# The first feature block of the first tile, computed in groups of 128 tokens between the pieces of the attention's lead-in

## The chip, the cores and the metric

The kernel runs on one core of one Trainium2 chip. The metric is the device time of one execution in microseconds (us). The kernel before took 1025.87 us, the median of 3 runs (1025.23 to 1028.19). A difference of a few tenths of a per cent is what such a measurement can tell from no change.

## The reference

All data is fp32. Three stages follow each other.

```python
# 1. attention in chunks of 32 tokens, 8 heads of 64, 768 tokens, 4 batches
for c in range(nc):
    k_full = np.concatenate([mem_k, k_ctx], axis=2)      # 8 memory + 16 left + 32 + 8 right = 64 keys
    scores = scale * np.matmul(q_c, k_full.transpose(0, 1, 3, 2))
    a = np.exp(scores - max); a = a / (sum(a) + 1e-09)
    out[:, :, c_start:c_end] = np.matmul(a, v_full)
x = out.transpose(0, 2, 1, 3).reshape(3072, 512)
# 2. first MLP: the largest of three projections, then one back
h = np.maximum(np.maximum(x @ w1, x @ w2), x @ w3)      # 512 -> 768
x = h @ w_out
# 3. second MLP
h = x @ w_in                                             # 512 -> 2048
g = np.where(h >= 1, h, np.where(h <= -1, 0.0, (h + 1) ** 2 / 4))
return g @ w_out2
```

## The kernel before

The 3072 tokens are cut into 8 tiles of 384 tokens (`TT`), and a tile into 3 groups of 128 (`GPT`). Phase A does attention and the first MLP, phase B the second MLP. Each engine has its own program, written out by hand; the order of work on an engine is the order of its program, and semaphores tie the engines together.

**Matrix products of the MLPs.** Each operand is split in two fp32r parts, `hi` and `lo`. The helper `three` (L399 to L404) issues three matmuls for one product: w_hi by x_hi (L402), w_lo by x_hi (L403), w_hi by x_lo (L404). Each loads its own weights of 128x128 and streams the tokens; in the first MLP that is 384 columns. In `layer1(t, a, f, w)` (L406) a feature block f of 128 features is made for one of the three weight matrices w, over 4 blocks of 128 input features (`KD`): 12 matmuls of 384 columns into the PSUM bank `mlp[w]`. A tile has 6 feature blocks, each for w = 0, 1, 2. ScalarE copies the bank of w = 0 (`h_first`), VectorE takes the maximum with the banks of w = 1 and w = 2 (`h_second`, `h_third`), and the result is split again (`h_high`, `h_low`).

**Attention of a group.** TensorE makes the scores (`scores`, L371, 64 small fp32 matmuls). VectorE takes the row maximum and subtracts it (`softmax_shift`), ScalarE takes the exponential, VectorE makes sums, reciprocal and product (`softmax_scale`), TensorE transposes the probabilities (`transposes`, L378, 4 matmuls with 128x128 weights and 128 columns), ScalarE copies them out (`transposed`), TensorE multiplies by V (`weighted_v`, L395, 64 small fp32 matmuls), ScalarE and VectorE split the result into `x_hi` and `x_lo` (`x_high`, `x_low`; semaphore `x_lo_done`).

**The lead-in.** Inside a loop the attention of the next tile's three groups is set between the feature blocks of this tile. Before the first tile there is nothing to set it between: TensorE does the attention of groups 0 to 2 alone (L472 to L486) and then begins `tile_a(0, ...)`, whose first `layer1` waits for the `x_lo` of all three groups (L457). After the 12 matmuls of w = 0 the scores of group 3 are made (L460), then w = 1 and w = 2 follow. In the first three groups the exponentials go to the banks `mlp[0]` to `mlp[2]` (`first_exponent`, L546), which are free again once `prob_done` has counted the group.

**Weights of phase A** come in 8 pieces of 768 KB through three staging buffers (`load_wa`, L227). ScalarE copies a piece to its `hi` part (`w_high`); the `lo` part is made by GpSimd for pieces 0 and 1 (L332 to L335, semaphore `wa_first`) and by VectorE for the others (`w_low`). A staging buffer is loaded again when its piece is split (L230). Piece f holds the weights of feature block f for w = 0, 1, 2. In ScalarE's program the split of piece 1 stands behind the `x_high` of group 2 (L608, L609).

Of the kernel before, what the change touches and what calls it, by code (L numbers as in the profile page):

```python
# [11 lines left out]
P = 128  # L12
# [15 lines left out]
GPT = TT // P  # L28
TOKENS = B * S
TILES = TOKENS // TT  # L30
KD, KF1, KF2 = DM // P, F1 // P, F2 // P
# [13 lines left out]
def build_attention_and_two_mlps(nc, qk_l, v_l, w123, w_out1, w_in2, w_out2, out):  # L45
# [8 lines left out]
    with ExitStack() as ctx:  # L54
        def psum(name, cols):
            return ctx.enter_context(nc.psum_tensor(name, [P, cols], F32))

        def sem(name):
            return ctx.enter_context(nc.semaphore(name))

        def sbuf(where, name, shape, dt=F32):
            return where.enter_context(nc.sbuf_tensor(name, [P, *shape], dt))
# [22 lines left out]
        w123_hi = sbuf(phase_a, "w123_hi", [KF1, 3 * KD, P], F32R)  # L85
        w123_lo = sbuf(phase_a, "w123_lo", [KF1, 3 * KD, P], F32R)
# [29 lines left out]
        x_hi, x_lo = (x0_hi, x1_hi), (x0_lo, x1_lo)  # L116
        y_hi, y_lo = (y0_hi, y1_hi), (y0_lo, y1_lo)

        mlp = [psum(f"mlp{i}", BANK)[:, :] for i in range(MLP_BANKS - 1)]
# [29 lines left out]
        sum_done, den_done, rec_done, prob_done = sem("sum_done"), sem("den_done"), sem("rec_done"), sem("prob_done")  # L149
        trans_done, prob_t_done = sem("trans_done"), sem("prob_t_done")  # L150
        attn_done, x_hi_done, x_lo_done = sem("attn_done"), sem("x_hi_done"), sem("x_lo_done")
        stage_a_in = [sem(f"stage_a_in{i}") for i in range(A_STAGES)]
        wa_hi_done, wa_first, wa_split = sem("wa_hi_done"), sem("wa_first"), sem("wa_split")
        mlp_done = sem("mlp_done")
# [23 lines left out]
        def h_wait(e, s, t, f):  # L178

            e.wait_ge(s, KF1 * t + f + 1)  # L180
# [5 lines left out]
        def weights_split(e, n):  # L186

            if n < A_FIRST:
                e.wait_ge(wa_first, n + 1)
            else:  # L190
                e.wait_ge(wa_split, n - A_FIRST + 1)
# [164 lines left out]
        def _(pe):  # L356
            def scores_ready(n, j, uses):

                pe.wait_ge(qk_in[j], 16 * (uses + 1))
                if not isinstance(n, int) or n:  # L360
                    pe.wait_ge(sub_done, n)

            def scores(j):

                q, k = q_of(j), k_of(j)
                for i in range(HALF_HEADS):
                    for c in range(CPG):
                        part = slice(c * CHUNK, (c + 1) * CHUNK)
                        for r in range(2):
                            rows = slice(r * D, (r + 1) * D)  # L370
                            last = pe.matmul(scores_v[part, r, i], q[rows, i, part], k[rows, i, c], start=True, stop=True)  # L371
                last.then_inc(scores_done, 1)

            def transposes(n, slot):

                pe.wait_ge(prob_done, n + 1)
                for m in range(HALF_HEADS):
                    last = pe.transpose(trans_v[:, m], prob[:, slot, 2 * m:2 * m + 2], ident[:, :])  # L378
                last.then_inc(trans_done, 1)

            def weights_ready(n, j, uses):

                pe.wait_ge(v_in[j], 16 * (uses + 1))
                pe.wait_ge(prob_t_done, n + 1)
                if not isinstance(n, int) or n:
                    pe.wait_ge(x_lo_done, n)

            def weighted_v(j):

                for m in range(2):  # L390
                    for c in range(CPG):
                        for r in range(2):
                            for i in range(2):
                                rows = slice(i * D, (i + 1) * D)
                                last = pe.matmul(attn_o[r * D:(r + 1) * D, i, m, c], v_raw[rows, j, 2 * m + r, c],  # L395
                                                 prob_t[rows, 2 * m + r, c], start=True, stop=True)
                last.then_inc(attn_done, 1)

            def three(out_ap, ab, first, last):  # L399

                a_hi, a_lo, b_hi, b_lo = ab
                pe.matmul(out_ap, a_hi, b_hi, start=first, stop=False)  # L402
                pe.matmul(out_ap, a_lo, b_hi, start=False, stop=False)  # L403
                return pe.matmul(out_ap, a_hi, b_lo, start=False, stop=last)  # L404

            def layer1(t, a, f, w, ahead=None):  # L406
                bank = mlp[w]
                if f:

                    h_wait(pe, (h_part_done, h_max2_done, h_max3_done)[w], t, f - 1)  # L410
                elif w < 2:

                    pe.wait_ge(y_copied, KD * t + 3 + w)
                if isinstance(t, int) and t == 0 and w == 0:
                    weights_split(pe, f)
                for k in range(KD):
                    if ahead is not None and k == KD - 1:
                        ahead()
                    last = three(bank[:, 0:TT], (w123_hi[:, f, KD * w + k], w123_lo[:, f, KD * w + k],
                                                 x_hi[a][:, k], x_lo[a][:, k]), k == 0, k == KD - 1)  # L420
                last.then_inc(mlp_done, 1)

            def layer2(t, a, d):
                bank = mlp[L2_BANK[d]]
                if d == 0:
                    if isinstance(t, int) and t == 0:
                        weights_split(pe, A_PIECES - 1)
                    h_wait(pe, h_max2_done, t, KF1 - 1)
                if d == KD - 1:
                    pe.wait_ge(y_copied, KD * (t + 1) + 1)  # L430
                for f in range(KF1):

                    if d == 0 and f in (0, KF1 - 1):
                        h_wait(pe, h_lo_done, t, KF1 - 2 if f == 0 else f)
                    wc = slice(f * DM + d * P, f * DM + (d + 1) * P)
                    last = three(bank[:, 0:TT], (w_out1_hi[:, wc], w_out1_lo[:, wc], h_hi[:, f], h_lo[:, f]),
                                 f == 0, f == KF1 - 1)
                last.then_inc(mlp_done, 1)

            def tile_a(t, a, attention, first=False):  # L440

                n0 = GPT * (t + 1)
                for f in range(KF1):
                    j, r = divmod(f, 2)

                    def ahead():
                        weights_ready(n0 + j, j, t + 1)
                        if j + 1 < GPT:
                            scores_ready(n0 + j + 1, j + 1, t + 1)

                    if attention and f == 0:
                        scores_ready(n0, 0, t + 1)
                    if attention and r == 0 and j:
                        weighted_v(j - 1)
                        scores(j)
                    if f == 0:
                        pe.wait_ge(x_lo_done, GPT * (t + 1))  # L457
                    layer1(t, a, f, 0)
                    if attention and f == 0:
                        scores(0)  # L460
                    if attention and r:
                        transposes(n0 + j, (a + 1 + j) % 2)
                    layer1(t, a, f, 1)
                    layer1(t, a, f, 2, ahead if attention and r else None)
                if attention:
                    weighted_v(GPT - 1)
                for d in range(KD):
                    layer2(t, a, d)
# [12 lines left out]
            transposes(1, 1)  # L481
            weights_ready(1, 1, 0)
            weighted_v(1)
            transposes(2, 0)
            weights_ready(2, 2, 0)
            weighted_v(2)  # L486
            tile_a(0, 0, True, True)
            with pe.Fori(0, B - 1) as b:
                tile_a(2 * b + 1, 1, True)
                tile_a(2 * b + 2, 0, True)  # L490
# [45 lines left out]
        def _(act):  # L536
            def copy(o, i):
                return act.activation(o, i, ACT.Copy)  # L538
# [11 lines left out]
            def w_high(n):  # L550
                act.wait_ge(stage_a_in[n % A_STAGES], 16 * (n // A_STAGES + 1))
                copy(first_weights(n)[0], stage_of(n)).then_inc(wa_hi_done, 1)

            def transposed(n):

                act.wait_ge(trans_done, n + 1)
                if not isinstance(n, int) or n:
                    act.wait_ge(attn_done, n)
                copy(prob_t[:, :, :, :], trans_c).then_inc(prob_t_done, 1)

            def x_high(n, x, j):
                act.wait_ge(attn_done, n + 1)
                copy(x_of(x_hi[x], j), attn_x).then_inc(x_hi_done, 1)
# [41 lines left out]
            transposed(1)  # L605
            x_high(1, 0, 1)
            transposed(2)
            x_high(2, 0, 2)  # L608
            w_high(1)  # L609
            tile_a(0, 0, range(A_FIRST, A_PIECES))  # L610
            with act.Fori(0, B - 1) as b:
                tile_a(2 * b + 1, 1)
# [246 lines left out]
```

## Time and profile before

| | |
|---|---|
| median of 3 runs | 1025.87 us (1025.23 to 1028.19) |
| the profiled execution, its time | 1025.81 us |
| the profiled execution, its span | 1024.0 us |
| TensorE busy (PE) | 1004.9 us, 98% of the span |
| VectorE, ScalarE, GpSimd busy | 412.6, 302.3, 48.9 us |
| first 25.6 us of the span (first slice of 40) | PE busy five tenths, DMA engines eight tenths |

The span runs from the first to the last instruction of the profiled execution; its time has 1.81 us more, which lies outside of the span. PE stands for the matmuls, PEld for the weight loads, which overlap them. The profile models the end of a matmul, so the step from the start of one to the start of the next says what it costs. The chain of waits is followed back from the last instruction to whatever released each one.

### The profile page before, as it was taken

What the parts mean: (1) busy time and instruction counts of PE and PEld (TensorE: products, weight loads), DVE (VectorE), ACT (ScalarE), POOL (GpSimd) and SP (SyncE); (2) the same over time, 40 slices, a digit from 0 to 9 for tenths busy, and PEclk for the clock granted to TensorE, in tenths of its full rate; (3) what the DMA queues carried; (4) which work ended last, traced back from release to release, by engine and by line L of the source; (5) the groups of instructions that cost most, each with busy time, mean ns of one, the idle gap of its engine ahead of it and who ended that gap; (6) DMA issues with size and microseconds to landing.
All of it is one profiled execution on the core that took longest, in us unless ns stands there. A gap on an engine that the chain in (4) does not pass through costs nothing.

```text
span 1024.0 us, 19464 instructions
## 1 busy us (share of the span) xinstructions
PE 1004.9 (98%) x8160; PEld 940.8 (92%) x8160; DVE 412.6 (40%) x757; ACT 302.3 (30%) x543; POOL 48.9 (5%) x44
## 2 busy tenths in 40 slices
PE   5999999999999999999999999999999999999998
PEld 4999999999999999999999999999999899999997
DVE  4552424143342524224543444434434344344343
ACT  3342222222221212244333323333233233332322
POOL 1100000000000000054500000000000000000000
PEclk9999999999999999999999999999999999999999
DMA  8452223122222310055300000010000000000000
GB/s 360 166 186 69 98 84 105 53 84 89 98 73 65 104 52 2 24 159 163 109 32 31 1 31 31 8 54 0 31 31 0 31 31 31 31 0 0 31 0 31
DMA packets 21950, 65.96 MB, mean 64 GB/s; under 512 B 2432, under 2 KB 6528, under 8 KB 21888
## 3 DMA queue, kind: packets, MB, share of 16 engines
q1 hardware_dynamic: 21888, 65.02, 18.4%
q8 instruction: 53, 0.87, 0.4%
q14 instruction: 9, 0.07, 0.0%
HBM read 52.43 MB, written 12.58 MB: 63 GB/s over the span
## 4 chain that ended last, share of the span: by engine, by line
PE 98%; issue 1%; DMA 0%; DVE 0%; ACT 0%
PE mlp L402 20%; PE mlp L404 20%; PE mlp L403 20%; PE scores_ps L404 6%; PE scores_ps L403 6%; PE scores_ps L402 6%; PE trans_ps L403 3%; PE trans_ps L404 3%; PE trans_ps L402 3%; PE attn_ps L395 3%; PE attn_ps L404 2%; PE attn_ps L402 2%; PE attn_ps L403 2%; PE scores_ps L371 2%; PE trans_ps L378 1%
## 5 line engine op out<-in xcount | busy, mean ns | idle before, releaser
L402 PE MATMUL mlp<-x_hi,w_hi 128*128 128x384 f32 x576 | 197.6, 343 | 3.7 <-ACT y_stage L538 2.1
L404 PE MATMUL mlp<-x_lo,w_hi 128*128 128x384 f32 x576 | 193.6, 336 | 0.0
L403 PE MATMUL mlp<-x_hi,w_lo 128*128 128x384 f32 x576 | 193.3, 336 | 0.0
L657 ACT ACTIVATE squared<-clamped,half_col 128x384 f32<-128x384 f32 x128 | 78.9, 617 | 257.5 <-DVE clamped L804 257.5
L402 PE MATMUL mlp<-y_hi,w_in_hi 128*128 128x384 f32 x384 | 129.2, 336 | 1.5 <-issue 1.5
L404 PE MATMUL mlp<-y_lo,w_in_hi 128*128 128x384 f32 x384 | 129.3, 337 | 0.0
L403 PE MATMUL mlp<-y_hi,w_in_lo 128*128 128x384 f32 x384 | 128.8, 336 | 0.0
L402 PEld LDWEIGHTS mlp<-x_hi,w_hi 128*128 128x128 f32 x576 | 108.7, 189 | 6.4 <-ACT y_stage L538 2.7
L403 PEld LDWEIGHTS mlp<-x_hi,w_lo 128*128 128x128 f32 x576 | 108.8, 189 | 0.0
L404 PEld LDWEIGHTS mlp<-x_lo,w_hi 128*128 128x128 f32 x576 | 108.7, 189 | 0.0
L808 DVE TENSOR_TENSOR g_lo<-g_f,g_hi 128x384 fp32r<-128x384 f32 x128 | 73.3, 573 | 81.6 <-ACT g_hi L538 81.6
L404 PE MATMUL scores_ps<-w_out_lo,g_hi 128*128 128x512 f32 x256 | 101.4, 396 | 0.0
L403 PE MATMUL scores_ps<-w_out_hi,g_lo 128*128 128x512 f32 x256 | 100.9, 394 | 0.0
L402 PE MATMUL scores_ps<-w_out_hi,g_hi 128*128 128x512 f32 x256 | 99.5, 389 | 0.0
L804 DVE TENSOR_SCALAR clamped<-mlp 128x384 f32<-128x384 f32 x96 | 53.4, 556 | 113.9 <-PE mlp L404 113.9
L538 ACT ACTIVATE g_hi<-g_f 128x384 fp32r<-128x384 f32 x128 | 67.3, 526 | 85.3 <-DVE g_f L806 85.3
L806 DVE TENSOR_TENSOR g_f<-squared,mlp 128x384 f32<-128x384 f32 x96 | 53.2, 555 | 65.6 <-ACT squared L657 65.6
L402 PEld LDWEIGHTS mlp<-y_hi,w_in_hi 128*128 128x128 f32 x384 | 72.1, 188 | 5.2 <-issue 1.8
L538 ACT ACTIVATE h_hi<-h_max 128x384 fp32r<-128x384 f32 x48 | 25.2, 524 | 173.8 <-DVE h_max L732 173.8
L403 PEld LDWEIGHTS mlp<-y_hi,w_in_lo 128*128 128x128 f32 x384 | 72.1, 188 | 3.4
L404 PEld LDWEIGHTS mlp<-y_lo,w_in_hi 128*128 128x128 f32 x384 | 72.0, 188 | 0.0
L726 DVE TENSOR_TENSOR h_max<-h_part,mlp 128x384 f32<-128x384 f32 x48 | 26.6, 554 | 112.4 <-PE mlp L404 112.4
(77 smaller groups left out, 1401.0 us busy)
## 6 DMA issues: line engine op xcount, KB each, us to landing
qk_raw<-qk_l SPq DMA_DIRECT2D x24, 768.0 KB, 4.8
v_raw<-v_l SPq DMA_DIRECT2D x24, 512.0 KB, 5.5
y_scratch<-y_stage SPq DMA_DIRECT2D x32, 192.0 KB, 1.9
y_raw<-y_scratch SPq DMA_DIRECT2D x8, 768.0 KB, 4.2
out<-out_stage SPq DMA_DIRECT2D x24, 256.0 KB, 2.0
stage_b<-w_in SPq DMA_DIRECT2D x16, 256.0 KB, 2.9
stage_b<-w_out SPq DMA_DIRECT2D x16, 256.0 KB, 2.8
stage_a<-w SPq DMA_DIRECT2D x4, 768.0 KB, 6.9
```

The lines of the kernel that those rows point to most:

```text
L371: last = pe.matmul(scores_v[part, r, i], q[rows, i, part], k[rows, i, c], start=True, stop=True)
L378: last = pe.transpose(trans_v[:, m], prob[:, slot, 2 * m:2 * m + 2], ident[:, :])
L395: last = pe.matmul(attn_o[r * D:(r + 1) * D, i, m, c], v_raw[rows, j, 2 * m + r, c], prob_t[rows, 2 * m + r, c], start=True, stop=True)
L402: pe.matmul(out_ap, a_hi, b_hi, start=first, stop=False)
L403: pe.matmul(out_ap, a_lo, b_hi, start=False, stop=False)
L404: return pe.matmul(out_ap, a_hi, b_lo, start=False, stop=last)
L538: return act.activation(o, i, ACT.Copy)
L657: act.activation(squared[:, f % 2], clamped[:, f % 2], ACT.Square, bias=half_col[:, 0:1], scale=0.5).then_inc(square_done, 1)
L726: dve.tensor_tensor(h_max[:, f % 2], h_part[:, :], mlp[1][:, 0:TT], ALU.max).then_inc(h_max2_done, 1)
L804: dve.tensor_scalar(clamped[:, f % 2], h, -1.0, 1.0, ALU.max, ALU.min).then_inc(clamp_done, 1)
L806: dve.tensor_tensor(g_f32[:, f % 2], squared[:, f % 2], h, ALU.max).then_inc(g_done, 1)
L808: dve.tensor_tensor(g_lo[:, f % G_RING], g_f32[:, f % 2], g_hi[:, f % G_RING].bitcast(F32), ALU.subtract).then_inc(g_split, 1)
```

## The change

A new helper `first_block(w, j)` computes feature block 0 of tile 0 for weight matrix w and for the 128 tokens of group j alone: the same 12 matmuls, with 128 columns each. The nine calls take the place of the three `layer1` of f = 0, which are left out of the first tile. Two of them are placed around the transposes of group 2, one behind the `weighted_v` of group 2, and six after that, with the scores of group 3 behind `first_block(0, 2)`. Each w = 0 call waits for the `x_lo` of its own group. In ScalarE's program the split of piece 1 is moved ahead of the `x_high` of group 2.

```diff
+            def first_block(w, j):
+
+                if w == 0:
+                    pe.wait_ge(x_lo_done, j + 1)
+                if j == 0:
+                    if w == 0:
+                        weights_split(pe, 0)
+                    pe.wait_ge(prob_done, w + 1)
+                tok = slice(j * P, (j + 1) * P)
+                for k in range(KD):
+                    last = three(mlp[w][:, tok], (w123_hi[:, 0, KD * w + k], w123_lo[:, 0, KD * w + k],
+                                                  x_hi[0][:, k, tok], x_lo[0][:, k, tok]), k == 0, k == KD - 1)
+                if j == GPT - 1:
+                    last.then_inc(mlp_done, 1)
...
+                    if first and f == 0:
+                        continue
...
             weighted_v(1)
+            first_block(0, 0)
             transposes(2, 0)
+            first_block(1, 0)
             weights_ready(2, 2, 0)
             weighted_v(2)
+            first_block(2, 0)
+            for w in range(3):
+                first_block(w, 1)
+            scores_ready(3, 0, 1)
+            first_block(0, 2)
+            scores(0)
+            first_block(1, 2)
+            first_block(2, 2)
             tile_a(0, 0, True, True)
...
             transposed(2)
+            w_high(1)
             x_high(2, 0, 2)
-            w_high(1)
             tile_a(0, 0, range(A_FIRST, A_PIECES))
```

## Rows read from the trace of the kernel before

**Rows 1.** The page: busy time of the engines, granted clock by slices, the chain by engine.

```profile
PE 1004.9 (98%) x8160; PEld 940.8 (92%) x8160; DVE 412.6 (40%) x757; ACT 302.3 (30%) x543; POOL 48.9 (5%) x44
...
PEclk9999999999999999999999999999999999999999
...
PE 98%; issue 1%; DMA 0%; DVE 0%; ACT 0%
```

**Rows 2.** Timeline of PE, 17 to 25.3 us: start, us, engine, line, operation, count, idle before.

```profile
19.31 1.11 PE L378 MATMUL trans_ps<-ident,prob 128*128 128x128 f32 x4
21.15 1.93 PE L395 MATMUL attn_ps<-prob_t,v_raw 64*64 64x32 f32 x64 [0.73 <-ACT prob_t L538]
24.67 0.66 PE L402 MATMUL mlp<-x_hi,w_hi 128*128 128x384 f32 x1 [1.59 <-issue]
25.13 0.52 PE L403 MATMUL mlp<-x_hi,w_lo 128*128 128x384 f32 x1
```

**Rows 3.** Timeline of PE, 28 to 30.6 us.

```profile
28.33 0.52 PE L404 MATMUL mlp<-x_lo,w_hi 128*128 128x384 f32 x1
28.78 1.19 PE L371 MATMUL scores_ps<-qk_raw 64*32 64x64 f32 x64
29.90 0.45 PE L402 MATMUL mlp<-x_hi,w_hi 128*128 128x384 f32 x1
30.18 0.34 PE L403 MATMUL mlp<-x_hi,w_lo 128*128 128x384 f32 x1
```

**Rows 4.** PE in narrow windows inside the transposes at 19.3 and 36.25 us.

```profile
19.31 0.69 PE L378 MATMUL trans_ps<-ident,prob 128*128 128x128 f32 x2
...
19.31 0.90 PE L378 MATMUL trans_ps<-ident,prob 128*128 128x128 f32 x3
...
36.25 0.38 PE L378 MATMUL trans_ps<-ident,prob 128*128 128x128 f32 x2
...
36.25 0.49 PE L378 MATMUL trans_ps<-ident,prob 128*128 128x128 f32 x3
```

**Rows 5.** Timeline of PE at 500 us: matmuls of 384 and 512 columns.

```profile
500.34 0.33 PE L404 MATMUL mlp<-y_lo,w_in_hi 128*128 128x384 f32 x1
500.52 0.39 PE L402 MATMUL scores_ps<-w_out_hi,g_hi 128*128 128x512 f32 x1
500.75 0.40 PE L403 MATMUL scores_ps<-w_out_hi,g_lo 128*128 128x512 f32 x1
```

**Rows 6.** Timeline of weight loads (PEld) at 24.6 and 29.9 us.

```profile
24.64 0.29 PEld L402 LDWEIGHTS mlp<-x_hi,w_hi 128*128 128x128 f32 x1 [1.70 <-issue]
24.81 0.33 PEld L403 LDWEIGHTS mlp<-x_hi,w_lo 128*128 128x128 f32 x1
...
29.90 0.19 PEld L402 LDWEIGHTS mlp<-x_hi,w_hi 128*128 128x128 f32 x1 [0.17 <-issue]
30.00 0.19 PEld L403 LDWEIGHTS mlp<-x_hi,w_lo 128*128 128x128 f32 x1
```

**Rows 7.** Timeline of ScalarE, 20 to 26 us.

```profile
20.46 0.60 ACT L538 ACTIVATE prob_t<-trans_ps 128x512 f32<-128x512 f32 x1 [0.43 <-PE trans_ps L378]
23.63 1.48 ACT L538 ACTIVATE w_hi<-stage_a 128x1536 fp32r<-128x1536 f32 x1
```

**Rows 8.** Timeline of GpSimd, and of VectorE up to the first feature block.

```profile
14.46 3.44 POOL L335 TENSOR_TENSOR w_lo<-stage_a,w_hi 128x1536 fp32r<-128x1536 f32 x1 [12.99 <-ACT w_hi L538]
25.19 3.46 POOL L335 TENSOR_TENSOR w_lo<-stage_a,w_hi 128x1536 fp32r<-128x1536 f32 x1 [7.28 <-ACT w_hi L538]
...
23.77 0.69 DVE L716 TENSOR_TENSOR x_lo<-attn_ps,x_hi 128x512 fp32r<-128x512 f32 x1 [3.02 <-ACT x_hi L538]
```

**Rows 9.** Timeline of VectorE, 30 to 36 us: the softmax of group 3, piece 2.

```profile
30.73 0.69 DVE L698 TENSOR_TENSOR score<-scores_ps,row_max 128x512 f32<-128x512 f32 x1
32.29 0.55 DVE L726 TENSOR_TENSOR h_max<-h_part,mlp 128x384 f32<-128x384 f32 x1 [0.87 <-PE mlp L404]
33.92 0.69 DVE L711 TENSOR_TENSOR prob<-prob,row_rec 128x512 f32<-128x512 f32 x1
```

## The prediction

> **What bounds the kernel now.** I read the page first: TensorE (PE) is busy 98% of the span, the others 40% and less, and 98% of the chain of waits is PE's own work [rows 1]. So the end moves by whatever PE's program gets longer or shorter, as long as nothing new makes it wait. Then I read the timeline of PE where the change is. Until 24.67 us PE does the attention of three groups, with two holes: 0.73 us before the sums of group 2, which wait for ScalarE's copy, and 1.59 us before the first layer, where the profile says only "issue" but the x_lo of group 2 is being made, which ends at 24.46 us [rows 2, 8]. From 24.67 us on PE streams without a hole worth naming. These two holes, 2.3 us, are all that the change can fill with waiting time.
>
> The third thing to see is the rate. In the first 12 matmuls of 384 columns a step is (28.33 - 25.13) / 10 = 0.320 us, which is 384 columns at 1.2 GHz. From 30.18 us to the transposes at 36.25 us there are 35 such matmuls (11, 12 and 12), so a step is 6.07 / 35 = 0.173 us, and it is about that at 500 us too [rows 2 to 5]. So PE is on its low level up to some point between 28.33 and 29.90 us and on its high one (2.4 GHz) after. The granted clock on the page reads full in every slice [rows 1]; it doesn't show this, and the steps decide. The rise came at most 5.2 us after the first 384-column matmul. The attention before it, over 15 us of small fp32 matmuls and transposes, had not raised it.
>
> **The change part by part.** Removed: 36 matmuls of 384 columns, 12 on the low level (3.84 us) and 24 on the high one (24 x 0.173 = 4.15 us). Added: 108 matmuls of 128 columns, each with its own load of 128x128 weights. The columns in all are the same; the weight loads are three times as many. All hangs on what a pair of load and matmul costs at 128 columns, and no fp32r pair of this size is in the trace.
>
> From below: 512 columns take 0.23 us a step, 384 take 0.173, so cost is in proportion to columns, and 128 would be 0.058 us on the high level and 0.107 on the low one, if loads stay hidden [rows 2, 3, 5]. From above: a pair costs no more than the 384-column one, 0.173 and 0.320 us. The nearest rows are the transposes, 128x128 weights with 128 columns. One more of them adds 0.90 - 0.69 = 0.21 us on the low level and 0.49 - 0.38 = 0.11 (0.108) on the high one [rows 4]. They are plain fp32, which speaks against carrying them over. But the fp32r loads point the same way: where PE starts afresh, the second load begins 0.17 us after the first on the low level and 0.10 to 0.11 us on the high one [rows 6]. A load seems to take that long, and under 384 columns it hides. I take 0.108 us on the high level and 0.19 on the low one, the middle of 0.17 and 0.21. A group block of 12 is then 2.28 us or 1.30 us.
>
> On that price the Trainium skill bears twice (TensorE: Matmul & The Clock Gate). Its section "LDWEIGHTS (loading the stationary operand)" gives a load as its columns over 1.2 GHz, whatever the rows, which is 0.107 us for 128 columns; it would give the high-level term that I use. Its section "Back-to-back issue gap" has about 81 ns for a sustained pair at 128 columns; the trace has no such pair. By it the result is one of the rivals below.
>
> The sum, step by step. The transposes of group 2 began at 19.31 us; there the first group block begins now. Its waits are met: piece 0 was split at 14.46 + 3.44 = 17.90 us [rows 2, 8], and the x_lo of group 0 is older. Low level: 19.31 + 2.28 = 21.59. Transposes, 4 x 0.21 = 0.85: 22.44. Second group block: 24.72. ScalarE's copy took 20.46 to 21.06 us, from 1.15 to 1.75 us after the transposes began [rows 7], so now it ends near 23.3, under that block: the hole of 0.73 us is filled. The sums of group 2, 1.9 us [rows 2]: 26.62. The x_hi and x_lo of group 2 need 1.4 us more and are wanted four blocks later: the hole of 1.59 us is filled too. The sums themselves began 3.5 us later than before, though, because 2 x 2.28 us now stand ahead of them.
>
> Then five group blocks up to `first_block(0, 2)`. I let the clock rise 5.2 us after the sums end, as before: 2.28 blocks on the low level, 2.72 x 1.30 = 3.5 us on the high: 35.35. The scores of group 3 cost 30.01 - 28.65 = 1.36 us between two streams (the load at 29.90 us ends, and the matmul begins to stream, near 30.01) [rows 3, 6]. Two more blocks, 2.59: 39.3 us. Before, the same point was 30.01 + 4.15 = 34.17 us. PE is 5.1 us later, and with PE as the whole chain so is the end: 1025.81 + 5.1 = 1030.9 us for the profiled execution. That execution lies 0.06 us from the median of 1025.87, so I say 1031 us. With 0.17 and with 0.21 on the low level the same walk gives +4.2 and +6.0.
>
> Edits that I cost at nothing. Piece 1 split sooner: the split on GpSimd ended at 28.65 us and feature block 1 used it at 34.2 us, so it was 5.5 us early already [rows 8]. In ScalarE's program `w_high(1)`, 1.48 us, now stands before the `x_high` of group 2; it runs from 23.3 to 24.8 us and is covered by the sums that end at 26.6; without that cover it would push x_hi, which still has 5 us of blocks ahead of its user. The split on GpSimd then ends near 28.3 us, as before, and SP's `load_wa(4)`, queued behind it with the loads of V and K after it, goes out at the same time as before. Feature blocks 1 and 2 come later on PE, so VectorE's and ScalarE's slack for piece 2 and for group 3 grows. The blocks' waits for `prob_done` cost nothing: the one for group 2, the last, was already met when its transposes began at 19.31 us.
>
> **The rivals.**
>
> *The small pair is cheap (not slower).* Fp32r weights load in the background and 128 columns cost 0.058 and 0.107 us. For: the steps of 384 and 512 columns show no term of their own for a load. Against: rows 4 and 6. Walk: sums end at 24.63, four blocks on the low level until 29.85, then 0.65 + 1.36 + 1.39: 33.24 us, 0.9 us earlier. It then meets a wait. The probabilities of group 3 need their scores, 1.45 us of row maximum and subtraction, the exponential, and 1.77 us from the end of the first maximum to the last product (32.84 to 34.61) [rows 9]: some 4.0 us after the scores end at 31.8. PE wants to transpose them at 33.24 + 2.08 = 35.3 and would get them at 35.8. Net -0.4: 1025.4 us. It decides where a pair costs under about 0.09 us on the high level. The skill's 81 ns, with 0.107 to 0.16 us on the low level, gives between -0.1 and +2.5 us; that lies on the same side of what can be told.
>
> *The clock rises early.* The dense stretch begins with the first group block at 19.31 us, and the level is high by about 24.5. With cheap pairs this gives 24.63 + 5 x 0.69 + 1.36 + 1.39 = 30.85, less the 0.5 us wait: -2.8 us, 1023.0 us; with my price +2.9. For: the kind of matmul that stood ahead of the rise begins 5 us sooner. Against: the transposes and sums around them never raised it.
>
> *The clock stays low through the whole block.* For: the small matmuls and transposes up to 23 us didn't raise it, and the blocks' matmuls are small too. Against: they are of the kind that stood ahead of the rise, only shorter. Then all nine blocks cost 2.28: 26.62 + 11.4 + 1.36 + 4.6 = 43.9, and feature block 1 still pays its 5.2 us on the low level (16 steps x 0.147 = 2.4 us): +12.2 us, 1038 us.
>
> *A small pair costs as much as a large one*, the upper bound: blocks of 3.84 and 2.08 us, +13.9 us, 1039.7 us. For it speaks nothing but that no row excludes it.
>
> **How the numbers follow.** Forecast (pair near 0.108, clock as before) 0.36, from +3 to +7 us: 1029 to 1033. Cheap pair 0.34, 1024.8 to 1028. Early clock 0.09. Clock low throughout 0.12. Large price 0.09. A measurement of this kernel can tell about 0.3%, 3.1 us, from no change. Slower by more: 0.33 of the forecast, 0.12, 0.09: 0.54. Within: 0.34, 0.03 of the forecast and 0.03 of the early clock: 0.40. Faster by more: 0.06, the early clock with cheap pairs. The range from 1024 to 1040 us takes in the cheap pair, the forecast, the low clock and the upper bound.
>
> **What would show it.** The step of the 128-column matmuls in `mlp`, at 20 us (0.19 or 0.107) and at 38 us (0.108 or 0.058). The first such matmul at 19.3 us and the sums of group 2 at about 24.7 us. The moment at which the step drops, near 32 us. The first matmul of feature block 1 at 39.3 us. No idle time before the transposes of group 3; some there would mean the cheap pair. Wrong would make it: a small step, or a level that is high before the sums of group 2.

## The result, and the profile after

The changed kernel takes 1041.83 us, the median of 6 runs (1039.22 to 1043.29), against 1025.76 us for the kernel before in as many: a ratio of 1.0146, 95% interval 1.0130 to 1.0162. By the ratio it is slower by some 15 us. The profiled execution took 1039.32 us with a span of 1037.5 us, 13.5 us more than before.

The page shows that TensorE is still the bound. Its busy time grew by 17.0 us, that of VectorE, ScalarE and GpSimd by less than a microsecond each [rows 1].

```profile
PE 1021.9 (98%) x8232; PEld 958.6 (92%) x8232; DVE 413.0 (40%) x757; ACT 302.6 (29%) x543; POOL 49.1 (5%) x44
...
PE 98%; DMA 0%; DVE 0%; ACT 0%; issue 0%
```

The timeline of PE of the changed kernel, where the group blocks are, and where they end (start, us, operation, weights, moving operand):

```profile
19.55 0.47 PE L402 MATMUL mlp<-x_hi,w_hi 128*128 128x128 f32 x1
...
21.74 0.41 PE L403 MATMUL mlp<-x_hi,w_lo 128*128 128x128 f32 x1
21.95 0.41 PE L404 MATMUL mlp<-x_lo,w_hi 128*128 128x128 f32 x1
22.17 1.07 PE L378 MATMUL trans_ps<-ident,prob 128*128 128x128 f32 x4
...
29.04 0.41 PE L403 MATMUL mlp<-x_hi,w_lo 128*128 128x128 f32 x1
29.25 0.41 PE L404 MATMUL mlp<-x_lo,w_hi 128*128 128x128 f32 x1
...
46.35 0.41 PE L403 MATMUL mlp<-x_hi,w_lo 128*128 128x128 f32 x1
46.56 0.41 PE L404 MATMUL mlp<-x_lo,w_hi 128*128 128x128 f32 x1
46.77 0.63 PE L402 MATMUL mlp<-x_hi,w_hi 128*128 128x384 f32 x1
```

The step of the small pairs is 0.213 us at 22 us, at 29 us and still at 46 us. It is the step of the transposes on the low level [rows 4], and it never falls. Feature block 1 starts at 46.77 us; before it was 34.17 us. And TensorE is on the low level there too, for the first 12 wide matmuls:

```profile
50.08 0.52 PE L403 MATMUL mlp<-x_hi,w_lo 128*128 128x384 f32 x1
50.40 0.52 PE L404 MATMUL mlp<-x_lo,w_hi 128*128 128x384 f32 x1
50.72 1.05 PE L378 MATMUL trans_ps<-ident,prob 128*128 128x128 f32 x4
51.43 0.57 PE L402 MATMUL mlp<-x_hi,w_hi 128*128 128x384 f32 x1
51.84 0.33 PE L403 MATMUL mlp<-x_hi,w_lo 128*128 128x384 f32 x1
52.01 0.34 PE L404 MATMUL mlp<-x_lo,w_hi 128*128 128x384 f32 x1
```

384 columns go at 0.320 us a step up to 50.4 us and at 0.17 from 51.84 us. The level rose 5.1 us after the first wide matmul. Before it had risen by 29.90 us, at most 5.2 us after the first wide matmul too [rows 3], and feature block 1 was all on the high level. The sums of group 3, behind feature block 1, start at 55.94 us instead of 40.97: 15.0 us late. Of that 1.5 us comes back by the end, in waits of TensorE that are shorter in this profiled execution. Two waits for `y_stage` inside phase A take 0.73 and 0.64 us instead of 1.21 and 0.91, one of 0.43 us that the kernel before has ahead of scores at 321 us is missing, and the one at the change to phase B takes 1.25 us instead of 1.47. Together that is 1.4 us, and it belongs to the execution rather than to the change: the changed kernel run again (d2, below) waits 2.0 us for `y_stage` and 1.98 us at the change to phase B, and its span of 1039.0 us is the whole 15.0 us longer.

Four of the six runs have a mean granted clock of 0.998 and took 1041.7 to 1043.3 us, and the two with 1.000 took 1039.2 and 1039.3, the profiled one among them, so the median of the six lies 2.5 us above it; the kernel b2, below, shows a trace with 0.998.

### The profile page after: what moved, and what is told of

Same layout as the page of the kernel before. It is cut to its first block, busy times and chain, and to the rows that moved or that the text cites. A ratio compares the mean times of both kernels' runs of the same rounds, so it can differ in the third digit from the quotient of the medians.

```text
span 1037.5 us, 19608 instructions
## 1 busy us (share of the span) xinstructions
PE 1021.9 (98%) x8232; PEld 958.6 (92%) x8232; DVE 413.0 (40%) x757; ACT 302.6 (29%) x543; POOL 49.1 (5%) x44
## 4 chain that ended last, share of the span: by engine, by line
PE 98%; DMA 0%; DVE 0%; ACT 0%; issue 0%
PE mlp L402 21%; PE mlp L404 20%; PE mlp L403 20%; PE scores_ps L404 6%; PE scores_ps L403 6%; PE scores_ps L402 6%; PE trans_ps L403 3%; PE trans_ps L404 3%; PE trans_ps L402 3%; PE attn_ps L395 3%; PE attn_ps L404 2%; PE attn_ps L402 2%; PE attn_ps L403 2%; PE scores_ps L371 2%; PE trans_ps L378 1%; DMA qk_raw<-qk_l 0%
## 5 line engine op out<-in xcount | busy, mean ns | idle before, releaser
L402 PE MATMUL mlp<-x_hi,w_hi 128*128 128x384 f32 (+1 forms) x600 | 208.7, 348 | 1.4 <-ACT y_stage L565 1.4
L404 PE MATMUL mlp<-x_lo,w_hi 128*128 128x384 f32 (+1 forms) x600 | 204.7, 341 | 0.0
L403 PE MATMUL mlp<-x_hi,w_lo 128*128 128x384 f32 (+1 forms) x600 | 204.4, 341 | 0.0
L402 PEld LDWEIGHTS mlp<-x_hi,w_hi 128*128 128x128 f32 x600 | 118.5, 197 | 4.1 <-ACT y_stage L565 2.0
L403 PEld LDWEIGHTS mlp<-x_hi,w_lo 128*128 128x128 f32 x600 | 118.6, 198 | 0.0
L404 PEld LDWEIGHTS mlp<-x_lo,w_hi 128*128 128x128 f32 x600 | 118.4, 197 | 0.0
```

## The experiments

**a1: ScalarE's order alone.**

```diff
             transposed(2)
+            w_high(1)
             x_high(2, 0, 2)
-            w_high(1)
```

> The kernel before with only ScalarE's order changed: w_high(1) ahead of x_high(2). Theory (the 128-column pairs are the whole cost): no change, 1025 to 1028 us, and the first 384-column matmul moves later by up to 1 us, since x_high(2) is wanted at once here and w_high(1) of 1.48 us starts at 21.1 us. Rival (the order of ScalarE and of the queues behind it costs): 3 us or more above the kernel before.

1026.34 us median (10 runs), ratio 1.0009 (0.9998 to 1.0020); the first 384-column matmul stands at 24.83 us, 0.15 later. That is no more than executions differ there: b2, which is the kernel before up to that point, has it at 24.82. This part costs nothing that can be told.

**a2: all nine group blocks where the wide ones stood.** The edit is against the changed kernel.

```diff
-            first_block(0, 0)
             transposes(2, 0)
-            first_block(1, 0)
             weights_ready(2, 2, 0)
             weighted_v(2)
-            first_block(2, 0)
-            for w in range(3):
-                first_block(w, 1)
             scores_ready(3, 0, 1)
-            first_block(0, 2)
+            for j in range(GPT):
+                first_block(0, j)
             scores(0)
-            first_block(1, 2)
-            first_block(2, 2)
+            for w in range(1, 3):
+                for j in range(GPT):
+                    first_block(w, j)
```

> All nine group blocks of 128 columns where the three wide ones stood, so that no hole of the lead-in is filled; the rest as in the changed kernel. Theory (each pair costs 0.213 us on the low level wherever it stands, and the clock doesn't rise among them): feature block 1 starts near 49.3 us, 2.5 us later than in the changed kernel, in all about 1042 us where the changed kernel profiled at 1039. Rival (the pairs are slow, or the clock low, because they are mixed with transposes and sums): the step falls to 0.107 us within 6 us of the first pair, feature block 1 near 41 us, about 1033 us.

1040.93 us (4 runs), ratio 1.0158 (1.0141 to 1.0175). Timeline of PE at the first pair, the last, and the rise:

```profile
23.00 0.47 PE L402 MATMUL mlp<-x_hi,w_hi 128*128 128x128 f32 x1
23.27 0.42 PE L403 MATMUL mlp<-x_hi,w_lo 128*128 128x128 f32 x1
...
47.18 0.41 PE L404 MATMUL mlp<-x_lo,w_hi 128*128 128x128 f32 x1
47.40 0.63 PE L402 MATMUL mlp<-x_hi,w_hi 128*128 128x384 f32 x1
...
49.42 0.46 PE L402 MATMUL mlp<-x_hi,w_hi 128*128 128x384 f32 x1
49.72 0.34 PE L403 MATMUL mlp<-x_hi,w_lo 128*128 128x384 f32 x1
```

24 us of small pairs with nothing between them but one set of scores leave the level low, and 2.3 us of wide ones raise it. So it is not the mixing with transposes and sums that keeps it low. Feature block 1 starts 0.6 us later than in the changed kernel, not 2.5: I had forgotten that the blocks of groups 0 and 1 don't wait for the x_lo of group 2 and fill the second hole here too. What the interleaving alone brings is then 0.6 us, read from one execution of each.

**a3: groups 0 and 1 together, 256 columns, then group 2.**

```diff
             weighted_v(2)
+            for w in range(3):
+                first_block(w, 0, 2)      # tokens 0 to 255
+            scores_ready(3, 0, 1)
+            first_block(0, 2, 3)          # tokens 256 to 383
+            scores(0)
+            first_block(1, 2, 3)
+            first_block(2, 2, 3)
```

> Groups 0 and 1 together, 256 columns, 36 pairs while x_lo of group 2 is made; then group 2 with 128 columns, 36 pairs. Load theory (a pair costs two cycles per column of the weights, 256 cycles, or its own columns if those are more): 256 columns cost 0.213 us on the low level like 128. Stream rival (short matmuls cost two cycles per streamed column): 0.427 us. For the clock: if length or dense streaming raises it, it rises within 6 us of the first of them and the 128-column ones after cost 0.107 us, feature block 1 near 36 us, about 1028 us; if it stays low, 22.95 + 36 x 0.213 + 1.36 + 36 x 0.213 = 39.7 us, about 1032 us.

1024.85 us (10 runs), ratio 0.9995 (0.9985 to 1.0004). Timeline of PE around the rise, and at the small pairs after it:

```profile
27.15 0.42 PE L402 MATMUL mlp<-x_hi,w_hi 128*128 128x256 f32 x1
27.36 0.41 PE L403 MATMUL mlp<-x_hi,w_lo 128*128 128x256 f32 x1
...
27.84 0.28 PE L403 MATMUL mlp<-x_hi,w_lo 128*128 128x256 f32 x1
27.96 0.28 PE L404 MATMUL mlp<-x_lo,w_hi 128*128 128x256 f32 x1
...
32.19 0.28 PE L403 MATMUL mlp<-x_hi,w_lo 128*128 128x128 f32 x1
32.30 0.27 PE L404 MATMUL mlp<-x_lo,w_hi 128*128 128x128 f32 x1
...
34.42 0.39 PE L402 MATMUL mlp<-x_hi,w_hi 128*128 128x384 f32 x1
```

256 columns cost 0.213 us on the low level and 0.12 on the high one, and 128 columns cost 0.213 (a2) and 0.11: on the low level the same, on the high one nearly. So halving the columns from 256 saves next to nothing, and what sets the step at 128 is not the streaming. At 256 it may be either: 384 columns take 0.320 us on the low level, and 256 at that rate would take 0.213. With 256 columns the level rises, 4.5 us after the first of them, and the 128-column pairs behind it keep it. I had expected about 1028 us with the level rising; it rose sooner than I had reckoned, feature block 1 starts at 34.42 us instead of near 36, and the kernel can't be told from the one before.

**a4: weights of 64 columns.**

```diff
-                    last = three(mlp[w][:, tok], (w123_hi[:, 0, KD * w + k], w123_lo[:, 0, KD * w + k],
+                    last = three(mlp[w][0:D, tok], (w123_hi[:, 0, KD * w + k, 0:D], w123_lo[:, 0, KD * w + k, 0:D],
```

> The changed kernel with weights of 64 columns (half of the output features) in the nine group blocks; the other 64 features of block 0 are left out. Load theory (the load of the weights sets the step, two cycles per column): the step falls from 0.213 to 0.107 us, the blocks take 11.5 us less, about 1030 us. Stream rival (128 streamed columns cost 256 cycles whatever the weights): step and time as in the changed kernel, 1039 to 1042 us.

1022.78 us (10 runs), ratio 0.9972 (0.9962 to 0.9981). Timeline of PE:

```profile
19.66 0.31 PE L404 MATMUL mlp<-x_lo,w_hi 128*64 128x128 f32 x1
19.76 0.31 PE L402 MATMUL mlp<-x_hi,w_hi 128*64 128x128 f32 x1
...
25.00 0.22 PE L404 MATMUL mlp<-x_lo,w_hi 128*64 128x128 f32 x1
25.06 0.22 PE L402 MATMUL mlp<-x_hi,w_hi 128*64 128x128 f32 x1
...
29.98 0.39 PE L402 MATMUL mlp<-x_hi,w_hi 128*128 128x384 f32 x1
...
32.62 0.66 PE L378 MATMUL trans_ps<-ident,prob 128*128 128x128 f32 x4 [0.32 <-DVE prob L738]
```

Half the weight columns, half the step: 0.107 us on the low level, 0.06 on the high one. So the load sets the 0.213 us of full weights. This does not show how long a load of 64 columns takes, since 128 streamed columns at the rate of the 384 take 0.107 us too. I expected 1030 us and got 7 less, because the level rises too, 2.8 us after the first pair. This is what a cheap pair, with the level rising early, would have given: feature block 1 at 29.98 us, and then the wait of TensorE for the probabilities of group 3, 0.3 us of idle, as the cheap-pair rival had it.

**d1: the same, but both halves,** the second written over the first. 216 pairs: as many weight columns as in the changed kernel, twice the streamed ones.

```diff
+                for half in (slice(0, D), slice(D, P)):
+                    for k in range(KD):
+                        last = three(mlp[w][0:D, tok], (w123_hi[:, 0, KD * w + k, half], ...
```

> The changed kernel with each 128-column pair made as two pairs with 64 weight columns each (216 pairs; the second half of the features is written over the first, so block 0 keeps 64 of its 128 features). The weight columns loaded are the same in number as in the changed kernel, the streamed columns twice as many. If the low level is what costs most there, and stands or falls with how densely matmuls stream: the level rises within 5 us of the first pair, a step is 0.107 us and then 0.062 us, about 6 to 8 us over the run with one half, 1029 to 1031 us, 11 us below the changed kernel with as much to load and more to stream. Rival (the price of loading alone makes the loss): 216 x 0.107 us as before, 1039 to 1042 us.

1028.12 us (10 runs), ratio 1.0019 (1.0007 to 1.0031). Timeline of PE:

```profile
20.60 0.31 PE L404 MATMUL mlp<-x_lo,w_hi 128*64 128x128 f32 x1
20.71 0.31 PE L402 MATMUL mlp<-x_hi,w_hi 128*64 128x128 f32 x1
...
24.44 0.22 PE L402 MATMUL mlp<-x_hi,w_hi 128*64 128x128 f32 x1
24.50 0.22 PE L403 MATMUL mlp<-x_hi,w_lo 128*64 128x128 f32 x1
...
36.83 0.39 PE L402 MATMUL mlp<-x_hi,w_hi 128*128 128x384 f32 x1
```

On the low level 216 x 0.107 us is what the changed kernel pays for its 108 pairs. The level is high by 24 us, 4.2 us after the first pair, feature block 1 starts at 36.83 us instead of 46.77, and the kernel is 12.8 us faster than the changed one beside it (1040.95, below).

**d2: the changed kernel again,** beside d1.

> The changed kernel once more, beside the others on one chip: 1039 to 1043 us; all nine blocks at 0.213 us a step, the rise some 2 to 6 us after the first 384-column matmul. If the rise falls among the small pairs instead, the low level is chance, and the time is near 1032 us.

1040.95 us (4 runs), ratio 1.0150 (1.0133 to 1.0168). The steps are as in the first trace, and the rise comes 5.1 us after the first wide matmul. With a2 that makes three traces in which the level stays low among the pairs, so it is no chance of one execution.

**b2: small pairs far behind the rise.** Feature blocks 3, 4 and 5 of the first tile, 324 pairs of 128 columns.

```diff
+                if isinstance(t, int) and t == 0 and f in (3, 4, 5):
+                    for j in range(GPT):
+                        tok = slice(j * P, (j + 1) * P)
+                        for k in range(KD):
+                            last = three(bank[:, tok], ..., x_hi[a][:, k, tok], x_lo[a][:, k, tok]), ...
```

> The kernel before with feature blocks 3, 4 and 5 of the first tile in groups of 128 columns (324 pairs in place of 108 matmuls of 384), far behind the rise of the clock. Load theory: the step is 0.107 us on the high level, 324 x 0.107 - 108 x 0.173 = 16 us more, about 1042 us, if the level holds. Clock theory (a stream of such pairs with full weights does not hold the high level either, as it did not raise it in the changed kernel): the step goes to 0.213 us within some us of the first of them and the cost is nearer 40 us, about 1065 us. Rival (the pair is only slow on the low level or beside the lead-in): 0.058 us a step, no change.

1044.47 us (4 runs), ratio 1.0160 (1.0138 to 1.0182). Three of the four have a mean clock of 0.998; the fourth took 1041.19 us, near the 1042 of the load theory. Timeline of PE at the end of the three blocks, 39 us after the first small pair:

```profile
87.94 0.27 PE L403 MATMUL mlp<-x_hi,w_lo 128*128 128x128 f32 x1
88.06 0.27 PE L404 MATMUL mlp<-x_lo,w_hi 128*128 128x128 f32 x1
```

The step is 0.11 us throughout. So the part of my clock theory that a stream of such pairs can't hold the high level fell: they hold it and don't raise it. The sums that follow start at 88.26 us against 70.96 before, and the first of the three blocks at 49.22 against 49.18: 17.3 us more, 5.8 us for each feature block. That is the price of the load alone.

This trace also has a mean clock of 0.998, and shows where that comes from: the first matmuls of phase B, and the window (busy us, count, granted clock, DMA) over them.

```profile
503.65 0.42 PE L402 MATMUL mlp<-y_hi,w_in_hi 128*128 128x384 f32 x1 [2.27 <-issue]
...
503.90:507.30 3.40, 3.40 (x12) 0.51 0.67 193
```

After a hole of 2.27 us between the phases the level was low for 3.4 us, which costs some 1.7 us. In the traces of the changed kernel and the one before, with holes of 1.25 and 1.47 us, it stayed high, and in d2 after 1.98. The length of the hole alone does not decide: in the trace of d1 it was 2.26 us, and the steps behind it are those of the high level, here and for the 3.6 us that I read:

```profile
488.35 0.41 PE L402 MATMUL mlp<-y_hi,w_in_hi 128*128 128x384 f32 x1 [2.26 <-issue]
488.60 0.34 PE L403 MATMUL mlp<-y_hi,w_in_lo 128*128 128x384 f32 x1
```

What else it takes stays open.

**b3: fill the hole with the scores.** From the kernel before, without group blocks.

```diff
             weights_ready(2, 2, 0)
             weighted_v(2)
+            scores_ready(3, 0, 1)
+            scores(0)
             tile_a(0, 0, True, True)
```

> The kernel before with only the scores of group 3 moved: they stand behind the sums of group 2, where the profile has a hole of 1.59 us, and no longer behind the first 12 matmuls. Theory (the hole can be filled with work that costs nothing more): 1.0 to 1.3 us less, near 1024.5 us; feature block 1 near 33.0 us. Rival (the x_lo of group 2 or the clock comes later by as much): no change.

1025.10 us median (12 runs) against 1026.39, ratio 0.9985 (0.9972 to 0.9997). Timeline of PE:

```profile
23.17 1.18 PE L371 MATMUL scores_ps<-qk_raw 64*32 64x64 f32 x64
24.67 0.69 PE L402 MATMUL mlp<-x_hi,w_hi 128*128 128x384 f32 x1 [0.32 <-DVE x_lo L718]
...
32.08 0.33 PE L402 MATMUL mlp<-x_hi,w_hi 128*128 128x384 f32 x1
```

The hole is filled but for 0.32 us, the first block starts where it did, and the 37th wide matmul, the first of feature block 1, comes at 32.1 us instead of 34.17. That is 2.1 us, more than the scores; the level rose 2.3 us after the first wide matmul here instead of about 5. I take that part for chance of this execution, whose 1022.63 us is the second shortest of the twelve; that the filled hole lets the level rise sooner is not excluded. The 1.3 us between the medians is about the price of the scores on the low level. Of the kernels that compute everything it alone is faster than the kernel before with an interval clear of 1, by 0.15%, which is at the edge of what can be told.

**c1: group-wise for w = 0 alone,** 256 columns and then 128, the rest wide.

```diff
             weighted_v(2)
+            first_block(0, 0, 2)
+            scores_ready(3, 0, 1)
+            first_block(0, 2, 3)
+            scores(0)
+            first_block(1, 0, 3)
+            first_block(2, 0, 3)
```

> The group-wise idea kept only where the hole is: for w = 0 groups 0 and 1 together (256 columns, 12 pairs from 23.1 us), then group 2 (128 columns, 12 pairs), then scores; w = 1 and 2 with 384 columns. Load theory: 12 x 0.213 + 12 x 0.213 on the low level until near 28 us, then 1.2 for the scores and 24 x 0.173: feature block 1 near 33.5 us, 0.7 us earlier than before, 1025 us. Rival (any 128-column pair keeps the clock low long enough to cost more than the hole): later than 34.2 us, over 1026 us.

1025.43 us (12 runs), ratio 0.9990 (0.9978 to 1.0002), not to be told from before. In its trace PE goes on with 384 columns at 28.27 us; 24 steps later feature block 1 begins, at 32.54 us, 1 us earlier than the theory had it, since the level rose 3.4 us after the first 256-column matmul. That is 1.6 us before the start in the kernel before, and little of it reaches the end: this execution has two waits ahead of scores, 0.46 and 0.75 us at 202 and 320 us, where the one before has 0.43. A few small pairs behind wide ones don't cost what 108 at the start do.

**c3: matmuls for nothing in the idle start.**

```diff
+            for i in range(8):
+                pe.matmul(trans_ps[:, 0:P], ident[:, :], ident[:, :], start=True, stop=True)
             scores_ready(0, 0, 0)
```

> The kernel before with 8 unused fp32 matmuls of the identity (128x128 weights, 128 columns, into trans_ps) in the 3.7 us in which TensorE waits for the first load; nothing reads them. Theory (the level follows how densely the array streams): plain fp32 makes several passes, 0.43 us each on the low level, the level is high by 5 to 6 us, and if it holds through the lead-in the sums and the first block are shorter: 3 to 5 us less, 1021 to 1023 us. Rivals: the level falls again in the sparse lead-in, no change; or fp32 pairs count as little as the transposes and it never rises early, no change, or the scores of group 0 start late by up to 1 us.

1028.99 us (12 runs), ratio 1.0018 (1.0007 to 1.0030), where I had expected 3 to 5 us less. Timeline of PE, and windows over it (stretch, length, busy us, count, granted clock, DMA share, GB/s):

```profile
1.62 3.75 PE L473 MATMUL trans_ps<-ident 128*128 128x128 f32 x16 [1.62 <-POOL ident L329]
5.31 1.19 PE L371 MATMUL scores_ps<-qk_raw 64*32 64x64 f32 x64
8.35 0.85 PE L371 MATMUL scores_ps<-qk_raw 64*32 64x64 f32 x64 [1.85 <-DVE score L700]
...
12.20 1.17 PE L371 MATMUL scores_ps<-qk_raw 64*32 64x64 f32 x64 [0.30 <-DVE score L700]
...
2.00:6.00 4.00, 4.00 (x67) 1.00 0.96 372
6.60:9.80 3.20, 0.85 (x64) 1.00 1.01 419
10.00:20.00 10.00, 7.55 (x201) 0.50 1.02 413
20.00:30.00 10.00, 7.46 (x116) 0.50 0.47 187
```

The 1.00 of the first window is not to be trusted, since the scores at 5.31 us take as long as on the low level. The level did rise: the same 64 small matmuls take 1.19 us at 5.31 us, 0.85 at 8.35 and 1.17 again at 12.20. It was high from about 6.5 us and fell again within 4 us, in which TensorE was busy 0.85 us; the attention's lead-in then ran at 0.50 and with the steps that it always had. All twelve runs have a mean clock of 0.990 or less, so this is no accident of one execution. The matmuls of the identity (16 in the profile for the 8 issued, 0.23 us each, with weights of 128 columns) and the scores behind them were enough for the rise, where 108 fp32r pairs at 0.213 us were not: a step as long as a load is not by itself the sign of a form that leaves the level low. The first wide matmul came at 25.40 us, 0.7 us later than before. The rest of the loss in this trace is in later waits of TensorE that the profile puts down to "issue": 0.84 and 0.83 us at 204 and 322 us, where before there is one of 0.43, and 2.16 instead of 1.47 us at the change to phase B. Why they are longer was not tried.

## Why the prediction was wrong

It had the direction right, and that the load sets the price of a pair, and missed the size, 5.1 us where 15 came. By its own steps:

1. *The bound.* Right: PE is the whole chain, and what it lost the kernel lost.
2. *The price of a pair.* Right on the high level: 0.11 us (b2, a3). On the low one I took 0.19, the middle of the transposes' 0.21 and the fresh loads' 0.17; it is 0.213, the upper end. The fresh load was no measure of a sustained one. Over 108 pairs this is 2.5 us. That the load sets it is shown by a3 (256 columns cost the same) and a4 (half the weights, half the step). Two figures were drawn from the Trainium skill, TensorE: Matmul & The Clock Gate. The 0.107 us of a 128-column load, by its section "LDWEIGHTS (loading the stationary operand)", agrees with the step on the high level here, 0.11 us, and not with the 0.213 us on the low one. The 81 ns of a sustained pair, in its section "Back-to-back issue gap", are not met by these fp32r pairs, which take 110 ns (b2).
3. *"I let the clock rise 5.2 us after the sums end, as before."* This is the step that failed. It carried a delay over from 384-column matmuls, whose step grows with their columns, to 128-column pairs, whose step is set by their loads. In the changed kernel the level stayed low for all 27 us of them, and rose 5.1 us after the first wide matmul. The rows for a doubt were there, the transposes and sums that hadn't raised it; I gave the rival 0.12. Why such pairs don't raise the level no run shows; the runs only part the forms that did from the one that did not.
4. *The rival "the clock stays low".* It is what happened. With its 0.19 it gave +12.2 us; with 0.213 the same walk gives 19.31 + 2.56 + 0.85 + 2.56 + 1.9 = 27.2, + 5 x 2.56 + 1.36 + 2 x 2.56 = 46.5 us for feature block 1 (measured 46.77, with a start 0.24 us later, at 19.55), + 2.4: +14.7 us, against 15.0 in the trace. The upper bound of the range, 1040 us, had been set with the level rising as before and so did not contain it.
5. *The holes.* The second was filled. The first was not wholly worth its 0.73 us: a2, which leaves it open, is 0.6 us later. ScalarE's order and piece 1: nothing, right (a1).

The 15 us in parts: 5.8 for the loads on the high level (b2's figure for one block); less about 2.2 for the two holes; the rest, near 11.4, is the low level. It can be worked out: 108 x (0.213 - 0.112) = 10.9 for the pairs, 12 x 0.147 = 1.8 and some 0.5 for feature block 1 and the transposes and matmuls after it, less 12 x 0.147 = 1.8 that the kernel before paid itself. And it was measured: d1, with the same loads and the level high 4.2 us after its first pair, starts feature block 1 9.9 us sooner, has it all on the high level, and is 12.8 us faster than the changed kernel.

## What to carry to other kernels

Cutting the moving operand of an fp32r matmul with 128 weight columns from 256 to 128 columns saved next to nothing here, since the load of the weights then sets the step: count weight columns as well as moving ones. Before work is moved into a stretch where TensorE is on its low level, ask whether that work can raise the level by itself, and measure it; these fp32r pairs of 128 by 128 did not. Of the ways tried to use the hole, the one that paid was to fill it with work that has to be done anyway, in the same form, as the scores in b3.

## What the runs showed of the hardware

- An fp32r pair with 128 weight columns costs 0.213 us on the low level with 128 and with 256 moving columns, and 0.11 and 0.12 on the high one (a2, a3, b2); with 64 weight columns and 128 moving ones 0.107 and 0.06 (a4, d1).
- Up to 108 pairs of 128 by 128, 24 to 27 us of them, didn't raise the level (the changed kernel, d2, a2); 324 of them over 39 us kept it once it was high (b2). Plain fp32 matmuls of the same size, 16 in the profile, and 64 small ones, 4.9 us in all, did raise it (c3). Pairs with 256 or 384 columns, or with 64 weight columns, raised it 2.3 to 5.6 us after the first (a2, b3, a4, c1, d1, a3, the changed kernel, a1).
- The level fell after a hole of 2.27 us in one execution (b2), for 3.4 us, and stayed high after one of 2.26 us in another (d1). Such a drop costs 1.7 us; that the runs with a mean clock of 0.998, some 2 us longer, have the same one is likely from the mean and not shown.
- The granted clock of a stretch can read 1.00 where the steps show 1.2 GHz, at the start of a trace: the kernel before up to its rise [rows 1, 2], and c3 up to 6.5 us. The steps decide.
